# Attention and two gated layers on one core: the local scores of both heads in one matmul over 128 rows, from the second batch on

## The reference

```python
# attention: B, H, S, D = 4, 8, 576, 64
q_d, k_d, v_d = (a.reshape(B, H, 144, 4, D).mean(axis=3) for a in (q, k, v))
out_up = np.repeat(sm_attn(q_d, k_d, v_d), 4, axis=2)     # softmax over 144 averaged positions
scores = scale * np.matmul(q, k.transpose(0, 1, 3, 2))
scores = np.where(abs(i - j) < 4, scores, -1e9)            # the local part: 7 keys for each query
out_local = softmax(scores) @ v
x = (out_up + out_local) as (2304, 512)
# first MLP: x (2304, 512), w1 and w2 (512, 1024), w3 (1024, 1024), w_out (1024, 512)
x = ((x @ w1) * (x @ w2)) @ w3 @ w_out
# second MLP: u1, u2, u3 (512, 768), u_out (768, 512)
y = np.maximum(np.maximum(x @ u1, x @ u2), x @ u3) @ u_out
```

## Time and profile before

| what | value |
|---|---|
| median of 3 runs | 684.14 us (682.67 to 686.3) |
| profiled execution | 683.57 us, span 681.8 us |
| TensorE busy | 671.7 us, 99% of the span |
| VectorE busy | 399.5 us, 59% |
| ScalarE busy | 268.4 us, 39% |
| GpSimd busy | 348.2 us, 51% |
| local score matmuls (L914) | 16 units of 96 records, first at 6.9 us, last at 238.3 us |

### The profile page before, as it was taken

The page is one execution under the profiler, slowest core; times in us unless marked ns, Lnnn a source line. Parts: engine busy times, 40 slices in busy tenths (PEclk is TensorE's granted clock), DMA queues, the critical chain, the costliest instruction groups (busy, mean ns, idle before and its releaser), DMA issues.

```text
span 681.8 us, 16896 instructions
## 1 busy us (share of the span) xinstructions
PE 671.7 (99%) x6848; PEld 642.7 (94%) x6848; DVE 399.5 (59%) x755; ACT 268.4 (39%) x590; POOL 348.2 (51%) x368
## 2 busy tenths in 40 slices
PE   8999999999999999999999999999999999999998
PEld 7778988999998999999999998999999999999998
DVE  4464654656676654367444464576576666656673
ACT  5565433433534344466545464122431223312221
POOL 6989667847964244455254434123571335904341
PEclk9999999999999999999999999999999999999999
DMA  9885488888957849967999598997399764997632
GB/s 312 266 290 154 130 227 253 246 281 240 271 149 221 255 132 376 342 221 259 333 356 367 185 364 286 415 370 253 122 396 346 233 247 150 344 367 246 236 120 92
DMA packets 91181, 178.21 MB, mean 261 GB/s; under 512 B 8161, under 2 KB 40161, under 8 KB 90337
## 3 DMA queue, kind: packets, MB, share of 16 engines
q1 hardware_dynamic: 91104, 177.14, 76.1%
HBM read 135.69 MB, written 41.42 MB: 260 GB/s over the span
## 4 chain that ended last, share of the span: by engine, by line
PE 87%; DMA 4%; DVE 3%; issue 2%; POOL 1%; ACT 1%; SPq 1%; DVEq 0%; ACTq 0%; POOLq 0%
PE psum L897 27%; PE psum L898 26%; PE psum L899 25%; PE psum L936 3%; DMA weights_stream<-attention 2%; PE psum L914 2%; PE psum L907 2%; PE psum L924 1%; PE psum L945 1%; DMA weights_split<-gate_weights_stream 1%; DMA attention<-ident 1%; POOL xy L1751 1%; DVE attention L1171 0%; POOL second_split L1692 0%; ACT attention L1466 0%
## 5 line engine op out<-in xcount | busy, mean ns | idle before, releaser
L1692 POOL TENSOR_TENSOR second_split<-xy,second_split 128x384 fp32r<-128x384 f32 x99 | 104.4, 1073 | 156.3 <-ACT second_split L1466 156.3
L897 PE MATMUL psum<-second_split,weights_split 128*128 128x384 f32 x402 | 134.9, 336 | 1.2 <-ACT xy L1466 1.2
L898 PE MATMUL psum<-second_split,weights_split 128*128 128x384 f32 x402 | 134.3, 334 | 0.0
L899 PE MATMUL psum<-second_split,weights_split 128*128 128x384 f32 x402 | 134.3, 334 | 0.0
L897 PE MATMUL psum<-weights_split 128*128 128x384 f32 x278 | 94.0, 338 | 0.4 <-ACT gate L1466 0.2
L899 PE MATMUL psum<-weights_split 128*128 128x384 f32 x278 | 92.9, 334 | 0.0
L898 PE MATMUL psum<-weights_split 128*128 128x384 f32 x278 | 92.9, 334 | 0.0
L1692 POOL TENSOR_TENSOR weights_split<-xy,weights_split 128x384 fp32r<-128x384 f32 (+1 forms) x65 | 74.1, 1156 | 19.8 <-ACT weights_split L1466 19.5
L897 PEld LDWEIGHTS psum<-second_split,weights_split 128*128 128x128 f32 x402 | 75.4, 188 | 2.7 <-ACT xy L1466 1.5
L898 PEld LDWEIGHTS psum<-second_split,weights_split 128*128 128x128 f32 x402 | 75.5, 188 | 0.0
L899 PEld LDWEIGHTS psum<-second_split,weights_split 128*128 128x128 f32 x402 | 75.5, 188 | 0.0
(11 more groups left out here) (143 smaller groups left out, 1398.2 us busy)
## 6 DMA issues: line engine op xcount, KB each, us to landing
weights_split<-weights_stream SPq DMA_DIRECT2D x39, 768.0 KB, 5.5
weights_split<-weights_stream SPq DMA_DIRECT2D x54, 512.0 KB, 6.5
weights_split<-gate_weights_stream SPq DMA_DIRECT2D x105, 256.0 KB, 4.7
weights_stream<-attention SPq DMA_DIRECT2D x48, 256.0 KB, 3.9
xy<-wa SPq DMA_DIRECT2D x40, 256.0 KB, 4.8
attention<-qk SPq DMA_DIRECT2D x16, 576.0 KB, 5.1
weights_stream<-attention SPq DMA_DIRECT2D x24, 384.0 KB, 3.7
weights_split<-weights_stream SPq DMA_DIRECT2D x6, 1152.0 KB, 5.0
```

What stands on the lines that cost most here:

```text
L897: pe.matmul(out, lhs[:, 0], rhs[:, 0], start=first, stop=False, skip_group_check=read_between)
L898: pe.matmul(out, lhs[:, 0], rhs[:, 1], start=False, stop=False, skip_group_check=read_between)
L899: return pe.matmul(out, lhs[:, 1], rhs[:, 0], start=False, stop=last, skip_group_check=read_between)
L1692: return pool.tensor_tensor(out, full, high.bitcast(F32), ALU.subtract)
```

## The change

From the second batch on (`u >= PAIRS`, 12 of the 16 units; the code calls them padded) `qk_sb` has three planes: q, k of the first head with zeros under it, and k of the second head with zeros above it. One matmul over all 128 rows then gives the scores of both heads for a window: 24 matmuls instead of 48, each with 64 moving columns (two runs of 32, one for each plane) instead of 32, on 128 rows instead of 64. Both heads' scores now lie in bank 4, by group and head.

For this
- k is loaded by two DMAs of 64 partitions each and q by one, three instead of one;
- the zeros are set twice by `memset` after unit 3, once for all, and TensorE waits for them at unit 4;
- `qk_sum` becomes three reductions instead of one;
- the third plane lies where `prob` was. For the first four units `prob` still uses it; later the scaled probabilities stay in PSUM and the transpose reads them there. So the load for unit 4 also waits until unit 3's probabilities are transposed (`local_turned`), and stands 6 positions later on SyncE;
- `qkd` now shares its place with `prob_d`, so that `qk_sum(u)` waits for `down_turned` of the unit before, not `down_scored`.

The core of the diff:

```diff
-        out += [(position("load_qk", u - 1), ("QK", u)), (position("load_v4", u - 1), ("V4", u)),
+        out += [(position("load_qk", u - 1) + (6 if u == PAIRS else 0), ("QK", u)), (position("load_v4", u - 1), ("V4", u)),
...
-        qk_sb = cut(2 * S).rearrange("p (a s) -> p a s", a=2)
-        qkd = cut(2 * SD).rearrange("p (a s) -> p a s", a=2)
+        qk_sb = cut(3 * S).rearrange("p (a s) -> p a s", a=3)
...
+        prob = qk_sb[:, 2, 0:2 * TG * TW]
+        prob_t = cut(2 * TG * TW)
+        qkd_or_prob = cut(DJ * SD)
+        qkd = qkd_or_prob[:, 0:2 * SD].rearrange("p (a s) -> p a s", a=2)
+        prob_d = qkd_or_prob.rearrange("p (j k) -> p j k", j=DJ)
...
+        score_by_group = bank(4)[:, 0:2 * TG * TW].rearrange("p (g h k) -> p g h k", g=TG, h=2)
+        def padded(u):
+            return u >= PAIRS
...
             def load_qk(u):
                 ge(sp, local_scored, u)
-                sp.dma_start(qk_sb, qk[u]).then_inc(qk_in, 16)
+                if u < PAIRS:
+                    sp.dma_start(qk_sb[:, 0:2, :], qk[u]).then_inc(qk_in, 16)
+                    return
+                if u == PAIRS:
+                    sp.wait_ge(local_turned, PAIRS)
+                sp.dma_start(qk_sb[:, 0, :], qk[u, :, 0, :]).then_inc(qk_in, 16)
+                for h in range(2):
+                    rows = slice(D * h, D * (h + 1))
+                    sp.dma_start(qk_sb[rows, 1 + h, :], qk[u, rows, 1, :]).then_inc(qk_in, 16)
...
+                if u == PAIRS:
+                    pe.wait_ge(zeros_set, 1)
                 for t in range(TG * TI):
                     g, i = t // TI, t % TI
+                    if padded(u):
+                        mm = pe.matmul(score_by_group[TW * i:TW * (i + 1), g, :, :], qk_sb[:, 0, Q0[t]:Q0[t] + TW],
+                                       qk_sb[:, 1:3, K0[t]:K0[t] + TW], start=True, stop=True)
+                        continue
...
             def qk_sum(u):
-                dve.wait_ge(qk_in, 16 * (u + 1))
-                ge(dve, down_scored, u)
-                dve.tensor_reduce(qkd, qk_sb.rearrange("p a (s j) -> p a s j", j=FACTOR), AX_X,
-                                  ALU.add).then_inc(qk_summed, 1)
+                dve.wait_ge(qk_in, qk_count(u))
+                ge(dve, down_turned, u)
+                four = qk_sb.rearrange("p a (s j) -> p a s j", j=FACTOR)
+                if padded(u):
+                    dve.tensor_reduce(qkd[:, 0, :], four[:, 0], AX_X, ALU.add)
+                    dve.tensor_reduce(qkd[0:D, 1, :], four[0:D, 1], AX_X, ALU.add)
+                    dve.tensor_reduce(qkd[D:P, 1, :], four[D:P, 2], AX_X, ALU.add).then_inc(qk_summed, 1)
...
+                if padded(u):
+                    dve.tensor_tensor(score, score, each_key(lrc, u), ALU.mult).then_inc(local_scaled, 1)
+                    dve.wait_ge(local_scaled, u + 1)
+                    dve.transpose(prob_t, score.rearrange("p g h k -> p (g h k)")).then_inc(local_turned, 1)
+                    return
...
+                if u == PAIRS - 1:
+                    dve.wait_ge(local_turned, PAIRS)
+                    dve.memset(qk_sb[D:P, 1, :], 0.0)
+                    dve.memset(qk_sb[0:D, 2, :], 0.0).then_inc(zeros_set, 1)
```

More of the change, by code:

```diff
@@ L532, in build, with score_l, by_rows, each_key @@
         dnb, dsum, drc = (cut(DJ) for _ in range(3))
-        lmax, lrc = (cut(2 * TG).rearrange("p (h g) -> p h g", h=2) for _ in range(2))
+        lmax, lrc = (cut(2 * TG) for _ in range(2))
         score_d = bank(6)[:, 0:DJ * SD].rearrange("p (j k) -> p j k", j=DJ)
-        score_l = psum[:, 512 * 4:512 * 6].rearrange("p (h c) -> p h c", h=2)[:, :, 0:TG * TW].rearrange(
+        score_by_head = psum[:, 512 * 4:512 * 6].rearrange("p (h c) -> p h c", h=2)[:, :, 0:TG * TW].rearrange(
             "p h (g k) -> p h g k", g=TG)
+        score_by_group = bank(4)[:, 0:2 * TG * TW].rearrange("p (g h k) -> p g h k", g=TG, h=2)
+        def padded(u):
+            return u >= PAIRS
+        def score_l(u):
+            return score_by_group if padded(u) else score_by_head
+        def by_rows(t, u):
+            return t.rearrange("p (g h) -> p g h", h=2) if padded(u) else t.rearrange("p (h g) -> p h g", h=2)
+        def each_key(t, u):
+            return by_rows(t, u).unsqueeze(3).to_broadcast([P, TG, 2, TW] if padded(u) else [P, 2, TG, TW])
+        def qk_count(u):
+            return 16 * min(u + 1, PAIRS) + 48 * max(u + 1 - PAIRS, 0)
+        def prob_of(u):
+            return prob_t.rearrange("p (g h q) -> p h g q", g=TG, h=2) if padded(u) else prob_t.rearrange(
+                "p (h g q) -> p h g q", h=2, g=TG)
         turned_d = psum[0:TD, 512 * 6:512 * 8].rearrange("p (k c) -> p k c", k=2)[:, :, 0:DJ * P]
@@ L542, in build @@
         dmax, dsum_eps = (bank(6)[:, DJ * (SD + i):DJ * (SD + i + 1)] for i in range(2))
-        lsum, lsum_eps = (bank(4)[:, 400 + 2 * TG * i:400 + 2 * TG * (i + 1)].rearrange("p (h g) -> p h g", h=2)
-                          for i in range(2))
+        lsum, lsum_eps = (bank(4)[:, 400 + 2 * TG * i:400 + 2 * TG * (i + 1)] for i in range(2))
         w12 = w12_t[:, :].rearrange("p (s f w k c) -> p s f w k c", s=2, f=F1, w=2, k=KD)
@@ L936, in values @@
                         mm = pe.matmul(bank(4 + i)[D * h:D * (h + 1), PV + TQ * g:PV + TQ * (g + 1)],
-                                       v_sb[rows, g, D * h:D * (h + 1)], prob_t[rows, h, g, own:own + TQ],
+                                       v_sb[rows, g, D * h:D * (h + 1)], prob_of(u)[rows, h, g, own:own + TQ],
                                        start=True, stop=True)
@@ L1173, in qk_sum @@
             def qk_sum(u):
-                dve.wait_ge(qk_in, 16 * (u + 1))
-                ge(dve, down_scored, u)
-                dve.tensor_reduce(qkd, qk_sb.rearrange("p a (s j) -> p a s j", j=FACTOR), AX_X,
-                                  ALU.add).then_inc(qk_summed, 1)
+                dve.wait_ge(qk_in, qk_count(u))
[5 more added lines that the diff above has]
+                    dve.tensor_reduce(qkd[D:P, 1, :], four[D:P, 2], AX_X, ALU.add).then_inc(qk_summed, 1)
+                else:
+                    dve.tensor_reduce(qkd, four[:, 0:2], AX_X, ALU.add).then_inc(qk_summed, 1)
             def down_max(u):
@@ L1188, in local_max @@
                 dve.wait_ge(local_scored, u + 1)
-                dve.tensor_tensor(score_l, score_l, mask.unsqueeze(1).to_broadcast([P, 2, TG, TW]),
-                                  ALU.add).then_inc(masked, 1)
+                score = score_l(u)
+                both = mask.unsqueeze(2).to_broadcast([P, TG, 2, TW]) if padded(u) else mask.unsqueeze(1).to_broadcast([P, 2, TG, TW])
+                dve.tensor_tensor(score, score, both, ALU.add).then_inc(masked, 1)
                 dve.wait_ge(masked, u + 1)
-                dve.tensor_reduce(lmax, score_l, AX_X, ALU.max).then_inc(lmax_ready, 1)
+                dve.tensor_reduce(by_rows(lmax, u), score, AX_X, ALU.max).then_inc(lmax_ready, 1)
                 dve.wait_ge(lmax_ready, u + 1)
-                dve.tensor_tensor(score_l, score_l, lmax.unsqueeze(3).to_broadcast([P, 2, TG, TW]),
-                                  ALU.subtract).then_inc(lmax_taken, 1)
+                dve.tensor_tensor(score, score, each_key(lmax, u), ALU.subtract).then_inc(lmax_taken, 1)
             def scale_down(u):
@@ L1207, in scale_local @@
                 dve.wait_ge(lexp_done, u + 1)
-                dve.tensor_reduce(lsum, score_l, AX_X, ALU.add).then_inc(lsum_ready, 1)
+                score = score_l(u)
+                dve.tensor_reduce(by_rows(lsum, u), score, AX_X, ALU.add).then_inc(lsum_ready, 1)
                 dve.wait_ge(lsum_ready, u + 1)
@@ L1213, in scale_local @@
                 dve.wait_ge(lrc_ready, u + 1)
[L1214 removed]
+                if padded(u):
[3 more added lines that the diff above has]
+                    return
+                dve.tensor_tensor(prob.rearrange("p (h g k) -> p h g k", h=2, g=TG), score, each_key(lrc, u),
                                   ALU.mult).then_inc(local_scaled, 1)
                 dve.wait_ge(local_scaled, u + 1)
[L1217 to L1218 removed]
+                dve.transpose(prob_t, prob).then_inc(local_turned, 1)
+                if u == PAIRS - 1:
+                    dve.wait_ge(local_turned, PAIRS)
+                    dve.memset(qk_sb[D:P, 1, :], 0.0)
+                    dve.memset(qk_sb[0:D, 2, :], 0.0).then_inc(zeros_set, 1)
             def x_out(u):
```

11 lines of the change are left out of this document (3 added, 8 removed).

## The result

| | changed kernel | kernel before, beside it |
|---|---|---|
| median (lowest to highest), 4 runs each | 691.81 us (690.63 to 692.41) | 683.84 us (682.67 to 686.3) |
| ratio, 95% interval | 1.0102 [1.0073, 1.0132] | |
| profiled execution, span | 692.2 us, 690.4 us | 683.57 us, 681.8 us |

The changed kernel is slower by 1.0% (7 us by the ratio; the two medians lie 8.0 us apart). The forecast was 686.0 and "no change"; the measured median lies 0.8 us above the top of the range.

What follows compares the result with a forecast made beforehand. TensorE, busy 671.7 of 681.8 us, was taken as the bound. Terms -2.4 + 3.2 + 1.05 = +1.85 on the profiled 683.57 us give 685.4, plus 0.57 for the median: 686.0 us, range 681 to 691.

Steps and rivals of the forecast that it cites:

- Part 1: Score matmuls of 12 units: 0.81 us a group instead of 0.96, with fewer stops; together -2.4 us.
- The term for the stops (0.6): Unexplained TensorE stops of 1.2 us inside the score matmuls: half goes with half the records, 0.6 us gained.
- Part 2: Unit 4's late load, once: sum and x_out(3) late, TensorE stands at the first MLP's first matmul, +3.2 us.
- The bound of 4.8: Upper bound in us on TensorE's stand from unit 4's late load; the lower bound was 1.9.
- The last rival: Longer stand near unit 4, more late sums or TensorE's clock falling: +6.0 us, 690.1 us; chance 0.18.
- Part 3: Three reductions and three loads every unit: hidden except before scores(13) and scores(11), together +1.05 us (0 to 4).
- +0.75 at `scores(13)`: Before scores(13): the longer sum runs straight into x_out(12), for which TensorE already waits; +0.75 us.
- At `scores(11)` 0.3: Before scores(11): load up to 0.9 us later and longer sum delay x_out(10) past the scores' start; +0.3 us.
- Part 4: Scores and transpose in PSUM, the down_turned wait, SyncE's two more issues a unit: cost nothing.

Runs made afterwards that it cites:

- e10: Changed kernel with the 24 wide matmuls reordered, the six of one tile one after the other: 707.99 us.
- e8: Changed kernel with each of the 24 wide matmuls streaming 32 of its 64 moving columns: 690.61 us.
- e13: Kernel before, unchanged, run again for a second trace: 683.22 us.
- e5: Kernel before with q and k of units 4 and on loaded by three DMAs instead of one: 686.7 us, ratio 1.0029.
- e2: Kernel before with only unit 4's load 6 positions later and waiting for unit 3's transpose: 687.54 us, ratio 1.0078.
- e1: Changed kernel with unit 4's load issued as early as before, the first four units' scaled probabilities staying in PSUM: 686.09 us, ratio 1.0042.
- e3: Kernel before with qk_sum as three reductions from unit 4 on, from the same single load: 684.79 us, ratio 1.0023.
- e12: Changed kernel, unaltered, run again for a second trace: 690.58 us.
- e4: Changed kernel, load of unit 4 still late, qk_sum(4) moved behind x_out(3) and the four product_low on VectorE: 686.89 us, ratio 1.0056.
- e6: e1 with qk_sum(13) moved ahead of two long subtractions on VectorE: 683.05 us, ratio 0.9981.
- e11: e6 with q and k loaded by two DMAs, one for each head, instead of three: 682.78 us, ratio 0.9991.
- e7: Kernel before with only qk_sum(13) moved ahead of two long subtractions on VectorE: 683.11 us, ratio 0.9993.

## Where the prediction was right and where it was wrong

**Part 1, right.** 0.81 us a group, as forecast. e10 shows that the overlap of tiles makes it, e8 that the columns count; that they alone set the price is not shown. The term for the stops (0.6) can't be checked to a few tenths: in the new groups of the changed kernel's two traces stops of 0.3, and of 0.1 and 0.4 us are left (groups over 0.81 us at full clock), e13 has 1.2 us of them as the earlier trace rows, so most of it went; but e5's 2.4 us says that their size isn't fixed.

**Part 2, the mechanism right, the size too small; here the forecast failed.** Landing, sum, `x_out(3)`, x_split, `product_high`, `product_low`, the first MLP's first matmul came in this order and with the distances told. The stand was put at 3.2 us and measured 5.3. Three items of the term: the issues of q and k took 0.96 and twice about 0.6 us, not 0.33 each, so the last went at 64.6 instead of 64.2; it landed 4.6 us after it, not 3.6, so that the sum began at 69.28 instead of 67.8; and TensorE was through with what it had by 69.25, where the working had 69.7. 1.5 + 0.1 (sum 2.2 instead of 2.1) + 0.45 is the 2.1 that lacked. The bound of 4.8 did not hold either.

The second failure is an omission: the sum priced the stand as if TensorE came back at full clock. +2.2 us followed in the first pair of traces and +1.3 in the second, with the clock at 0.50 up to about 80 us. The last rival had named it, with a chance of 0.18; its mechanism came here, and its 690.1 is nearest to the 691.8 measured. That the totals lie so close is partly luck: it has nothing for the 2.6 us of late products, and 3 us for late sums or the clock together. e2 shows both, stand and clock, without any other part of the change, and e1 shows them by their absence.

**Part 3.** +0.75 at `scores(13)` was +0.9, right; e3 makes it by the sums alone. The clock behind it was again not counted (the other 1.4 of the 2.3 us lost there in the profiled execution; e12 kept its clock and lost 0.8 in all). At `scores(11)` 0.3 was forecast and nothing came: the sums began at 178.34, which is 173.36 plus the 4.7 us that TensorE was late by and 0.3, not plus 0.9, and `x_out(10)` ended just before TensorE was ready.

**Part 4, right.** The transposes from PSUM take 584 ns; the memsets fell into idle time (0.54 us each):

```profile
L1268 DVE STREAM_TRANSPOSE attention<-psum 128x384 f32<-128x384 f32 x11 | 6.4, 584 | 0.4
```

**What no step had.** 2.6 us at 511 and 599 us (2.8 in e12 against the same trace of before, 2.3 against e13), long after the last unit. The paired products of every trace, against the first trace of before, lose between 505 and 600 us:

| changed kernel and its variants | kernel before and its variants |
|---|---|
| after 2.6, e12 2.8, e1 3.1, e4 3.0, e6 2.7, e8 3.0, e10 2.7, e11 2.0 | e13 0.5, e2 -0.5, e3 1.0, e5 0.6, e7 0.9 |

So in these traces the sum of both places tells the two kinds apart, whether the load of unit 4 is late or early (e1), the sum of unit 13 late or early (e6), the loads three or two (e11), the columns 64 or 32 (e8). A single place does not: e3 loses 1.5 us at 599, e7 0.75 at 511, more than e11 there. The late load, the three sums and the three loads alone (e2, e3, e5) don't make it. No run took the new layout of `attention`, the probabilities in PSUM and the wait for `down_turned` without the new matmuls, so what in the new form matters was not tested.

The step just before the stops is the landing of the stores, as said above. Their 24 issues land after 6.8 to 7.0 us in the median in the eight traces of the new form, and after 5.9 to 6.2 in the six of the old one, the first trace of before with 6.0. ScalarE's waits for them are 9.7 and 11.8 us in the two traces of the changed kernel, 3.8 and 3.9 in those of before, though e3 and e5 have 9.7 and 8.6 too. Why stores of the same data land 0.8 us later, 250 us after 12 units of other score matmuls, is open; no run here was made on it.

By the first pair: -0.5, the stand 5.3, its clock 2.2, less 2.6 from 74 to 204 us, 2.3 at `scores(13)`, less 1.2 up to 268, 0.5 up to 505, 2.6 at the late products: 8.6, the growth of the span.

## What to carry to other kernels

When a load is moved behind a new condition, follow not its consumer but all that the in-order engine has queued behind that consumer: e4 cut a stand from 5.3 to 1.5 us with the load as late as ever. Price a stand of TensorE of several microseconds with the half clock behind it, 1.3 to 2.6 us here after 3.7 to 5.6. Small matmuls on tiles of 32 columns gain only while neighbours in the program use different tiles: 0.81 us against 2.22 for the same 24. And read a stop put down to "issue" against the waits written in the kernel: the two late products were waits for ScalarE and so for a store.

## What the runs showed of the hardware that was not expected

- The granted clock of TensorE (1.00 is 2.4 GHz, 0.50 is 1.2 GHz) fell to 0.50 in every stand of 3.7 to 5.6 us (the changed kernel twice, e2, e8, e10), and in e5 in the stop of 2.4 us. After the wait of 1.9 us at `scores(13)` (2.1 in e8) it fell in the changed kernel, e1, e3, e4, e8 and e10 and not in e12. After 1.5 us (e4) and 1.0 us (before) it did not, but neither did it after waits of 1.9 and 2.0 us near 415 us in e6 and e4. So the length of the wait alone doesn't decide it, and e4's expectation, which called 2.3 us too short, finds no support: e5's window behind 2.4 us reads

```profile
225.00:227.00 2.00, 1.76 (x55) 1.69 (x55) 0.90 (x2) 0.00 (x0) 1.87 (x2) 0.50 0.08 27
```

- Issuing a load on SyncE's queue right behind another one takes longer: 0.96 to 1.20 us for q or q and k behind `v_down` and some 0.6 for each half of k, where the same queue shows 0.33 when nothing was issued just before. Half the size lands sooner, a quarter does not land sooner still: 5.1 us after issue for 576 KB, 3.6 for 288 KB on 128 partitions, 4.0 for 144 KB on 64 (and 4.4 for e11's 288 KB on 64):

```profile
attention<-qk SPq DMA_DIRECT2D x12, 288.0 KB, 3.6
attention<-qk SPq DMA_DIRECT2D x24, 144.0 KB, 4.0
```

- A reduction costs by elements of a partition, not by partitions: 749 ns on 128 partitions (the row), 734 and 749 on 64. Split in three, a sum of 1152 elements of 1338 ns takes 2.2 us:

```profile
L1223 DVE TENSOR_REDUCE attention<-attention 128x144 f32<-128x576 f32 x11 | 8.2, 749 | 9.0 <-DMA attention<-qk 7.2 <-PE psum L968 1.8
```
